# Fused attention and mixture-of-experts kernel: key rounding head by head, two POOL steps exchanged, and the order of the last routing steps with six unread matrix products

## The reference

```python
scores = scale * np.matmul(q, k.transpose(0, 1, 3, 2))          # 2 x 8 heads, 576 x 576, dim 64
kth = np.partition(scores, -top_k, axis=-1)[..., -top_k:-top_k + 1]
scores = np.where(scores >= kth, scores, -1000000000.0)
attn = np.exp(scores - np.max(scores, axis=-1, keepdims=True))
attn = attn / (np.sum(attn, axis=-1, keepdims=True) + 1e-09)
x = np.matmul(attn, v)                       # reordered to 1152 tokens x 512
h = x @ w_in                                 # 512 x 2048
g = np.maximum(h, 0.0) + alpha * np.minimum(h, 0.0)
x2 = g @ w_out
logits = x2 @ w_gate
noisy = logits + np.log1p(np.exp(x2 @ w_noise)) * noise
# the two best of 8 experts for each token, softmax of the two as weights
out[mask] += top2_w[mask, k, None] * (np.maximum(x2[mask] @ w1[e], 0.0) @ w2[e])
```

## Time and profile before

| | us |
|---|---|
| median of 3 runs | 725.3 |
| lowest, highest | 724.16, 725.45 |
| the profiled execution's own time | 723.99 |
| its span in the trace | 722.2 |

### The profile page before, as it was taken

How to read it: one execution, slowest core, us unless ns; L and a number is a source line. 1 busy time by engine, 2 the same in 40 slices (tenths; PEclk the granted TensorE clock), 3 DMA queues, 4 the chain that set the end, 5 groups by cost and what they waited for, 6 DMA issues and landing times.

```text
span 722.2 us, 13742 instructions
## 1 busy us (share of the span) xinstructions
PE 660.5 (91%) x4688; PEld 563.1 (78%) x4688; DVE 528.7 (73%) x1111; ACT 466.6 (65%) x880; POOL 390.9 (54%) x436
## 2 busy tenths in 40 slices
PE   2468779999989999999999999899999999999994
PEld 2356657878867888888888788788998989989893
DVE  6999999989669989898998453785455554555520
ACT  6788877786887787787777645755354454544511
POOL 3598998878788677678767757121130311303112
PEclk9976999999999999999999999999999999999998
DMA  9889537545408535264472787745845828457222
GB/s 287 361 264 385 168 148 266 196 162 186 191 17 280 194 132 184 111 262 162 153 256 78 312 320 257 266 161 173 271 120 187 249 88 274 131 174 241 71 33 36
DMA packets 39964, 141.01 MB, mean 195 GB/s; under 512 B 11152, under 2 KB 12176, under 8 KB 35856
## 3 DMA queue, kind: packets, MB, share of 16 engines
q1 hardware_dynamic: 35520, 130.25, 50.2%
q0 software_dynamic: 4384, 9.98, 6.2%
HBM read 113.70 MB, written 45.73 MB: 221 GB/s over the span
## 4 chain that ended last, share of the span: by engine, by line
PE 70%; POOL 14%; ACT 6%; issue 4%; DVE 3%; DMA 2%; SPq 0%; POOLq 0%; ACTq 0%; DVEq 0%
PE bank L1275 11%; PE bank L1091 10%; PE ps_scores L1259 10%; PE bank L1054 7%; PE bank L1259 6%; PE bank L1030 6%; POOL expo L1778 4%; PE bank L1280 4%; PE bank L1059 3%; PE bank L1012 3%; PE ps_scores L981 3%; POOL w_in_parts L1790 2%; POOL k_parts L1735 2%; PE bank L1071 2%; PE bank L1294 1%
## 5 line engine op out<-in xcount | busy, mean ns | idle before, releaser
L443 DVE MAX8 top<-rest 128x8 f32<-128x576 f32 x216 | 152.3, 746 | 0.0
L1938 POOL DMA_INDIRECT out_dram<-ye,xe x24 | 42.8, 1784 | 189.9 <-ACT ye L1676 164.5
L1778 POOL TENSOR_TENSOR expo<-scores,expo 128x576 f32<-128x576 f32 x72 | 103.6, 1440 | 61.1 <-ACT scores L1368 61.0
L455 DVE MATCH_REPLACE8 rest<-top,rest 128x576 f32<-128x576 f32 x144 | 105.8, 742 | 0.0
L1091 PE MATMUL bank<-w_out_high,g_parts 128*128 128x512 f32 x288 | 99.6, 406 | 1.0 <-DVE g_parts L662 1.0
L669 DVE TENSOR_TENSOR w_lo<-raw,w_hi 128x1024 fp32r<-128x1024 f32 x64 | 78.0, 1225 | 20.0 <-ACT w_hi L1605 18.9
L1275 PE MATMUL bank<-w_hi,he_t 128*128 128x512 f32 x224 | 80.6, 401 | 0.0
L1030 PEld LDWEIGHTS bank<-v,prob_t 128*64 128x64 f32 (+1 forms) x1440 | 56.5, 143 | 28.8 <-ACT prob_t L1395 14.4
L1030 PE MATMUL bank<-v,prob_t 128*64 128x65 f32 (+1 forms) x1440 | 72.0, 239 | 4.6 <-ACT prob_t L1395 4.6
L1605 ACT CAST w_hi<-raw 128x1024 fp32r<-128x1024 f32 x64 | 66.7, 1045 | 6.7 <-DMA raw<-w_dram 6.5
L1259 PE MATMUL ps_scores<-xe_t,w_hi 128*128 128x320 f32 x320 | 70.9, 309 | 0.0
(11 more groups left out here) (242 smaller groups left out, 1622.6 us busy)
## 6 DMA issues: line engine op xcount, KB each, us to landing
raw<-w_dram SPq DMA_DIRECT2D x64, 512.0 KB, 9.7
w_in_parts<-w_parts_dram SPq DMA_DIRECT2D x14, 2048.0 KB, 7.9
x_sorted_dram<-x_sorted_dram SPq DMA_DIRECT2D x7, 2570.0 KB, 11.4
w_parts_dram<-w_in_parts SPq DMA_DIRECT2D x4, 2048.0 KB, 10.3
q_raw<-q_rows_dram SPq DMA_DIRECT2D x18, 256.0 KB, 4.9
w_in_raw<-w_in_dram SPq DMA_DIRECT2D x4, 1024.0 KB, 11.5
w_out_raw<-w_out_dram SPq DMA_DIRECT2D x4, 1024.0 KB, 14.2
w_lo<-w_parts_dram SPq DMA_DIRECT2D x2, 2048.0 KB, 13.1
```

The source lines that it names most:

```text
L443: nc.vector.max(dst, src).then_inc(chain if r < ROUNDS - 1 else dve_top, 1)
L455: nc.vector.match_replace(rest[:, k, :], top[:, (n + k) % 4, 8 * r:8 * r + 8], src, LOWEST).then_inc(chain, 1)
L1778: nc.gpsimd.tensor_tensor(expo[:, n % 4, :], scores[:, n % SBUFS, :], expo[:, n % 4, :], ALU.mult).then_inc(pool_prob, 1)
```

## The change

1. **The key tables.** Before, ScalarE rounds heads 0, 1, 2, 4, 6 ahead of the score copy of tiles 22, 24, 29, 30, 31 and heads 3, 5, 7 at the end of tiles 29, 30, 31. After, heads 0, 1, 2, 3, 4, 6 stand at the end of tiles 22, 24, 28, 29, 30, 32, and heads 5 and 7 ahead of the score copy of tiles 31 and 33. On POOL heads 2 to 7 move to tiles 29, 30, 31, 31, 32 and 33; before they stood at 30, 30, 31, 31, 32 and 32.
2. **`normalise` ahead of `low_g`** on POOL, in every block from the second on.
3. **The end, chunks 2 and 3 of block 8.** On ScalarE the rounding of chunk 2 and the ReLU of chunk 3 stand between the Exp and the Ln of block 7's softplus; `last_high_g(3)` and one weight piece stand ahead of `gap_exp`. On VectorE `last_low_g(2)`, `last_prelu(3)`, `last_low_g(3)` stand ahead of `score_tokens` of block 7, weight piece 0 ahead of `last_prelu(2)`, piece 1 ahead of `place_block`, and `weights_of` behind it.
4. **TensorE's end.** `rank(1)` stands behind the fourth `second_layer` of block 8, in the bank `ps_pt`. `x2_transpose` stands ahead of `block_at_slots(0)`, whose second half stands behind `gates`. Four products of 128x512 whose results nobody reads stand ahead of `rank(2)`, two behind it. The first scatter of block 7 waits for `weights1` in place of `slots1`.

```diff
-K_HIGH_AT = {22: 0, 24: 1, 29: 2, 30: 4, 31: 6}
-K_HIGH_BEHIND = {29: 3, 30: 5, 31: 7}
-K_LOW_AT = {24: 0, 26: 1, 30: 2, 31: 4, 32: 6}
-K_LOW_BEHIND = {30: 3, 31: 5, 32: 7}
+K_HIGH_AT = {31: 5, 33: 7}
+K_HIGH_BEHIND = {22: 0, 24: 1, 28: 2, 29: 3, 30: 4, 32: 6}
+K_LOW_AT = {24: 0, 26: 1, 29: 2, 30: 3, 31: 4}
+K_LOW_BEHIND = {31: 5, 32: 6, 33: 7}
...
-                if c == 2:
-                    score_tokens(EARLY, EARLY + 1, 1)
                 last_low_g(c)
                 if c == 1:
                     low_x2(0, x2_again[:, 0:MODEL])
+                    low_weights(0, 0, 1)
             last_prelu(3)
+            last_low_g(3)
+            score_tokens(EARLY, EARLY + 1, 1)
             pick_experts(EARLY, EARLY + 1, 1)
-            last_low_g(3)
+            low_weights(1, 0, 2)
+            place_block(EARLY, 1, ps_pt)
             weights_of(EARLY, EARLY + 1, 1, x2_first[0][:, WEIGHT:], x2_again[:, WEIGHT:])
-            place_block(EARLY, 1, ps_pt4)
             step(v3.tensor_scalar(slots_ahead, slots_row, base[:, 0:1], None, ALU.subtract))
-            for c in range(4):
+            for c in range(2, 4):
                 low_weights(c, 0, c + 1)
...
-            pe.wait_ge(act_gate, j)
-            rank(1, ps_pt4)
             second_layer(j, 3)
+            pe.wait_ge(act_relu, 4 * BLOCKS)
+            rank(1, ps_pt)
...
+            x2_transpose(j, ps_t, chunks=4 * j + 4)
+            pe.wait_ge(act_gate, j)
+            block_at_slots(0, range(2))
+            gates(j, ps_h[:, 0:2 * EXPERTS], x2_t.rearrange("p (k n) -> p k n", k=MK))
+            block_at_slots(0, range(2, MK))
+            early_rows()
+
+            def keep_clock(n):
+
+                for _ in range(n):
+                    pe.matmul(ps_y[:, :], w_out_high[:, 0:P], w_out_high[:, 0:MODEL], start=True, stop=True)
+
+            pe.wait_ge(act_x2_last, 1)
+            keep_clock(4)
             pe.wait_ge(route, mark["placed1"])
-            block_at_slots(0, range(2))
-            x2_transpose(j, ps_t, chunks=4 * j + 4)
-            block_at_slots(0, range(2, MK))
-            gates(j, ps_h[:, 0:2 * EXPERTS], x2_t.rearrange("p (k n) -> p k n", k=MK))
-            early_rows()
-            pe.wait_ge(act_relu, 4 * BLOCKS)
             rank(2, ps_pt)
+            keep_clock(2)
             block_at_slots(1)
...
                 act.wait_ge(route_act, 4 * turn + 1)
                 nc.scalar.activation(part, part, ACT.Exp, scale=-1.0).then_inc(route_act, 1)
+                if between:
+                    between()
                 act.wait_ge(route_act, 4 * turn + 2)
                 nc.scalar.activation(part, part, ACT.Ln, bias=1.0).then_inc(route_act, 1)
...
-            softplus(EARLY, EARLY + 1, 1)
-            last_high_g(j, 2)
-            last_relu_both(j, 3)
+            def third_and_last_chunk():
+                last_high_g(j, 2)
+                last_relu_both(j, 3)
+
+            softplus(EARLY, EARLY + 1, 1, between=third_and_last_chunk)
+            last_high_g(j, 3)
+            high_weights(1, 0, 0)
             gap_exp(EARLY, EARLY + 1, 1)
-            last_high_g(j, 3)
...
+                    if mlp and h == (1 if after_mixed else 0):
+
+                        normalise(blk - 1, 0)
+                    if mlp and h == 1 and blk > 1:
+                        normalise(blk - 1, 1)
                     if rest and h in REST_LOW_AT:
                         low_g(blk - 2, REST_LOW_AT[h])
...
-            pool.wait_ge(route, mark["slots1"])
+            pool.wait_ge(route, mark["weights1"])
             scatter(0, EARLY, x2_first[0])
```

More of the change, by code:

```diff
@@ L1496, in copy_gates, with softplus @@
                 nc.scalar.copy(dst, src).then_inc(act_gate, 1)
-            def softplus(a, b, turn, src=None):
+            def softplus(a, b, turn, src=None, between=None):
                 part = noisy[:, a:b, :]
@@ L1634, in _ @@
             last_relu_both(j, 2)
-            softplus(EARLY, EARLY + 1, 1)
-            last_high_g(j, 2)
-            last_relu_both(j, 3)
+            def third_and_last_chunk():
[4 more added lines that the diff above has]
+            high_weights(1, 0, 0)
             gap_exp(EARLY, EARLY + 1, 1)
-            last_high_g(j, 3)
-            for c in range(1, 4):
-                high_weights(c, 0, 0)
+            high_weights(2, 0, 0)
             copy_x2(j, last=True)
             copy_x2_t(j, x2_t, ps_t)
+            high_weights(3, 0, 0)
             softplus(j, j + 1, 2, ps_h[:, EXPERTS:2 * EXPERTS])
@@ L1834, in one_block @@
                         low_g(blk - 1, LOW_AT[h])
-                    if mlp and h == (1 if after_mixed else 0):
-                        normalise(blk - 1, 0)
-                    if mlp and h == 1 and blk > 1:
-                        normalise(blk - 1, 1)
                     if rest and h in REST_PRELU_AT:
@@ L1848, in one_block @@
                             pool.wait_ge(pool_g, 4 * (blk - 1) + PRELU_AT[h] + 1)
+                        elif h in REST_LOW_AT:
+                            pool.wait_ge(pool_g_low, 4 * (blk - 2) + REST_LOW_AT[h] + 1)
                         else:
```

## The result

| | before | changed |
|---|---|---|
| median, us | 725.3 | 728.49 |
| lowest, highest | 724.05, 726.12 (9 runs) | 726.71, 731.72 (9 runs) |
| ratio over all runs, 95% interval | | 1.0052 [1.0035, 1.0069] |
| profiled execution's own time, span | 723.99, 722.2 | 729.63, 727.9 |

The account below looks back on a forecast made before the run. TensorE was taken as the bound, holding 70% of the chain that ended last. Tile 17 -1.2, keys +5.8 and end -1.2 summed to +3.4 us on the median of 725.3: 728.7 us, range 724.0 to 731.5.

Parts of the forecast that it names:

- Neither sign of a wrong prediction: Wrong if POOL's product 33 follows its `prelu` within 3 us, or tiles 32 to 35 take no longer than before.
- Tile 17, -1.2: With `normalise` ahead of `low_g`, TensorE's 1.31 us wait for `x` goes: -1.2 us, between -1.3 and 0.
- the key term: Tiles 28 to 34, moved key roundings: +4.6 us of delay plus 1.2 of clock, +5.8, from +4.6 to +7.6.
- Up to tile 32, +0.9: POOL's product 32 ends at 204.2 against 203.3, behind head 5's remainder, so TensorE takes it 0.9 us later.
- Tile 33, +2.9: POOL waits for head 6's rounding, so TensorE starts tile 33 at 214.4 instead of 211.53, idle 3.7 us.
- One of the two waits that were to vanish here, the 0.28: Tile 32: with ScalarE ahead, TensorE's waits of 0.28 and of 1.39 us for `h_sb` were to vanish.
- Tile 34, +4.6 without the clock: POOL waits for head 7's rounding, so TensorE starts tile 34 at 222.6 instead of 218.05: +4.6 us in all.
- The clock, +1.2: Half clock behind the 3.7 us idle at tile 33 adds 1.2 us on the path, between 0 and +3.0.
- The rival of two falls: Tile 34's 2.0 us wait brings another clock fall, on 12 dense `second_layer` products: 730.5 us, chance 0.15.
- the kind clock: No clock fall behind the new waits and none at tile 25: 725.8 us, no change to measure, chance 0.15.
- The end, -1.2: From block 8's chunks 2 and 3 to item 0's third part: -1.2 us, bounds -2.0 and +1.7.
- No drain at the table load: End, ScalarE's table change: no 1.38 us drain counted; with it the end would give 0 in place of -1.2.

Follow-up runs that it names:

- The exchange alone: Kernel before with POOL's `normalise` moved ahead of `low_g` and nothing else: 0.9971 of the kernel before, -2.1 us.
- filled kernel: Changed kernel with 6, 10 and 7 unread TensorE products ahead of its waits for POOL's products 32, 33, 34: 1.0042, run again 1.0031 of the kernel before.
- the changed kernel again: Changed kernel, nothing altered, measured once more in the fourth comparison: 1.0043 of the kernel before, +3.1 us.
- The end alone: Kernel before with only the end's changes on VectorE, TensorE, ScalarE and the scatter's wait: 0.9983 of the kernel before, -1.2 us.
- old-keys kernel: Changed kernel with the key tables and POOL's wait as before: 0.9947 of the kernel before, -3.9 us; run again 0.9950, -3.6 us.
- head 6 early: Changed kernel with head 6 rounded ahead of tile 32's score copy instead of behind its exponentials: 0.9989 of the kernel before, -0.8 us.
- heads 6 and 7 early: Changed kernel with head 6 rounded ahead of tile 32's score copy, head 7 behind tile 32's exponentials: 0.9962 of the kernel before, -2.8 us.
- keys only: Kernel before with the new key tables and the POOL wait that goes with them: 1.0082 of the kernel before, +6.0 us.
- no unread products: Changed kernel without the six unread products around `rank(2)`: 1.0052 of the kernel before, +3.8 us.
- second comparison: Second of four sets of runs, each with its own kernel before, which took 730.2 us here; the last three used three different chips.

## Why the prediction was right

728.7 was predicted and 728.49 measured, and slower by over 0.2% had a chance of 0.70. The mechanism is the one foretold, but part of the closeness is luck. The change without its key tables gave 3.6 and 3.9 us where the sum has 2.4, and the tables cost 6.7 where it has 5.8: two misses of about a microsecond with opposite signs. The second is well within the noise, the first at the edge of it, and some 0.6 of both is the gain of `x` at tile 33, which the sum books with the keys. Neither sign of a wrong prediction came: POOL's product 33 starts 5.8 us behind the end of its `prelu`, and tiles 32 to 35 take longer in every trace with the new tables unchanged. Point by point:

- **Tile 17, -1.2.** By stages, tiles 14 to 26, with a fall of the clock in both: 72.03 to 70.80, -1.2. Tile 25, where 0 was put, gives nothing: TensorE's product with the values starts 66.71 us behind tile 14 before and 65.52 after, the same 1.2. The exchange alone gave -2.1; of that 0.6 lies at tile 33 and was counted inside the key term (the wait of 0.41 for `x` left out there), the rest of the difference is within the interval.
- **Up to tile 32, +0.9.** 35.28 to 36.22, +0.94.
- **Tile 33, +2.9.** TensorE starts it 117.19 us behind tile 14 in place of 115.49; with the 1.23 gained ahead of it that is +2.9. The idle time was foretold at 3.7 and is 4.04 where the clock did not fall in tile 32. POOL was to wait from 207.2 to 211.45, 4.2; it waited 4.44. One of the two waits that were to vanish here, the 0.28, is not among; it is this row of TensorE in the trace of before:

```profile
204.40 0.40 PE L981 MATMUL ps_scores<-k_parts,q_high 128*128 128x288 f32 x1 [0.28 <-ACT scores L1334]
```

- **Tile 34, +4.6 without the clock.** In the two traces of the filled kernel tiles 26 to 35 take 60.44 and 60.68 against 55.88 in the kernel before: +4.6 and +4.8. POOL's wait for head 7, foretold at some 2 us, is 2.29 in both. In the four traces with a fall at tile 33 it is 2.96 to 4.00, and with it grows the time from TensorE's start of tile 33 to ScalarE's copy of `x`, which stands ahead of head 7's rounding: 2.4 us without a fall, 3.1 to 4.1 with one. That is how the half clock gets through to product 34. Both steps of the replay, head 6 behind the exponentials and head 7 behind `copy_x_t` and the signs, stand in the rows of ScalarE above.
- **The clock, +1.2.** The filled kernels say 0.7 to 0.9, uncertain by some 2 us. The profiled execution had three falls in tiles 32 to 35, not one, and 2.9 us between 24.21 and 27.15; it lies 1.1 above its median. Two more traces of the same order in these tiles, the changed kernel again and the one without unread products, have one fall each and lie 0.6 and 1.6 us above 24.21. The rival of two falls, 730.5, is close to this execution and to the highest times (731.72); the kind clock is close to the trace of the changed kernel run again (no fall at tile 25, one at tile 33, 726.0 us). So these two look less like rivals than like the spread of one kernel, though no trace of the highest executions shows it. The step that I did not see is the fall in tile 32, behind a wait of 1.65 us.
- **The end, -1.2.** In the traces, from `rank(0)` to item 0's third part: 428.26 to 472.28 is 44.0, 434.85 to 477.41 is 42.6, -1.5. The end alone measured -1.2. One sign did not come: the interval from the fourth `second_layer` to item 0's third part was to shrink by about 1 us. From the start of the last product of that layer (459.51 before, 464.62 after) it is 12.8 us in both; all of the gain lies ahead of it. The prediction's own times, 1.3 earlier at the fourth layer and 1.2 at the third part, say so too, so the sign was worded wrongly and the term was not. Low parts of chunks 2 and 3 ended within 0.3 us of where the replay had them. `rank(2)` was given a lead of 0.65 and has 0.5. The replay already had the four unread products as the last thing ahead of it, 0.55 us behind VectorE's result; VectorE was ready 0.4 earlier than I had it, so they hold it longer. What they may pay back is the clock in item 0, which fell in the one trace without them.
- **No drain at the table load.** The Trainium skill ("ScalarE: Activation LUTs", What ACT_TABLE_LOAD costs) has a drain of 1.38 us at each change of table. The trace does not agree with the page here. ScalarE's timeline in the old-keys kernel, run again, which has the new end:

```profile
449.94 0.59 ACT L1453 ACTIVATE pos<-bank 128x512 f32<-128x512 f32 x1
450.55 1.28 ACT L1522 ACT_TABLE_LOAD   x1
451.84 0.21 ACT L1522 ACTIVATE noisy<-noisy 128x8 f32<-128x8 f32 x1
```

The step ahead of the load ends at 450.53 and the one behind it starts when the load ends, so nothing stands on either side, and the sum was right to leave the drain out.

What stays open is how much of the median is clock: the falls differ from execution to execution, and a trace is of one.

## What to carry over

When a step is moved to where its engine has room, ask first what that place waits for. Head 6's rounding was put on ScalarE in a tile where ScalarE runs ahead, but behind steps that wait for POOL, while POOL waits for the rounding: a wait of 4.4 us came in where there had been none, and one entry of a table took most of it out. Compare traces by stages between fixed points rather than from the start of the span, and read the clock's falls as spread of one kernel before they are read as an effect. Where a product is added to keep the clock up, look at whether the engine is already asked for by then; here, as far as the times can tell, it cost about as much as it kept.

## What the runs showed of the hardware

**The same idle time does not always bring a fall.** TensorE's wait at tile 32 is 1.63 to 1.65 us in six traces. In three of them the clock fell to 0.50 behind it (changed, head 6 early, heads 6 and 7 early), in three it stayed (keys only, no unread products, changed run again). A wait of 4.04 us at tile 33 brought a fall in all three traces that have it. At tile 25 a wait of 1.83 to 1.85 us went with a fall in three traces of seven, one of 1.25 us in one of three. There the traces with a fall take 1.4 to 1.7 us more than those without: 72.03 against 70.45 and 70.48 in the old order of POOL, 70.65 to 70.82 against 69.14 to 69.26 in the new. When part of the loss lies under a wait it can cost less: one fall at tile 33, seen from 213 to 217 us, took 0.6 us (24.21 to 24.83), a longer one there, seen from 211 to 219 us, took 1.6 (to 25.85).

**Stops in the straight code of the end on one chip.** In the second comparison all four traces have TensorE idle 3 to 5 us in about 448 to 458 with no engine behind it, or behind a ScalarE that stopped itself (`issue` and `remote` in the brackets mean that the profile names no instruction as the releaser). TensorE, then ScalarE, of the old-keys kernel:

```profile
451.94 1.11 PE L1072 MATMUL bank<-ident,expo 128*128 128x128 f32 x4 [3.46 <-issue]
```

```profile
443.39 0.59 ACT L1501 COPY expo<-bank 128x512 f32<-128x512 f32 x1 [1.58 <-remote]
...
445.53 0.60 ACT L1453 ACTIVATE neg<-bank 128x512 f32<-128x512 f32 x1 [1.55 <-remote]
```

The same program on another chip has neither; from `rank(0)` to the span's end it took 298.4 us on the one and 292.2 on the other. There is no trace of the kernel before from that chip, but its 730.2 us there, 5 to 6 more than elsewhere, fit the same stops. What the engines waited for no trace names, and it was not tried. One candidate is instruction fetch: the Trainium skill ("Runtime: NRT & Kernel Launch", Instruction fetch mechanics) has each engine's instructions come in by DMA in large blocks, read ahead in order. No run here shows that this was late.
